# One maximum unit of thirteen half passes moved from the place in front of the eighth score unit to that in front of the seventh

## What is computed

```python
q_pool = q.reshape(B, H, S // factor, factor, D).mean(axis=3)     # B=4, H=8, S=1152, D=64, factor=2
scores = scale * np.matmul(q_pool, k.transpose(0, 1, 3, 2))
scores = scores - np.max(scores, axis=-1, keepdims=True)
attn = np.exp(scores)
attn = attn / (np.sum(attn, axis=-1, keepdims=True) + 1e-09)
return np.matmul(attn, v).astype(np.float32)
```

## Time and profile before

| | |
|---|---|
| time, median of 3 runs (lowest, highest) | 917.2 us (916.99, 917.43) |
| the profiled execution, its own time | 918.22 us |
| span of that execution | 916.2 us |
| outside the span | 2.0 us |
| PE, PEld busy | 884.3 us (97%), 717.6 us (78%) |
| DVE, ACT, POOL busy | 545.8 us (60%), 470.6 us (51%), 387.3 us (42%) |
| granted TensorE clock, mean of the span | 0.995 |

### The profile page before, as it was taken

The page is one execution under the profiler, slowest core; times in us unless marked ns, Lnnn a source line. Parts: engine busy times, 40 slices in busy tenths (PEclk is TensorE's granted clock), DMA queues, the critical chain, the costliest instruction groups (busy, mean ns, idle before and its releaser), DMA issues.

```text
span 916.2 us, 18068 instructions
## 1 busy us (share of the span) xinstructions
PE 884.3 (97%) x7190; PEld 717.6 (78%) x7190; DVE 545.8 (60%) x971; ACT 470.6 (51%) x1017; POOL 387.3 (42%) x269
## 2 busy tenths in 40 slices
PE   4899999999999999998999999999999999999996
PEld 3566666676676666665999999999999999999733
DVE  6878888888888888853664434433433443443423
ACT  3677787877777777686543322322332332322202
POOL 3979999999999999997000000000000000000000
PEclk9999999999999999999999999999999999999998
DMA  7121122222212211303320000200000000476998
GB/s 237 39 75 55 51 79 79 79 79 78 69 63 80 79 50 56 97 1 117 115 69 1 1 1 0 93 1 1 1 1 1 1 1 1 168 244 219 302 369 286
DMA packets 47828, 76.42 MB, mean 83 GB/s; under 512 B 3584, under 2 KB 33408, under 8 KB 47744
## 3 DMA queue, kind: packets, MB, share of 16 engines
q1 hardware_dynamic: 47744, 75.26, 24.5%
HBM read 70.53 MB, written 4.72 MB: 82 GB/s over the span
## 4 chain that ended last, share of the span: by engine, by line
PE 54%; issue 26%; POOL 16%; DVE 2%; ACT 1%; DMA 0%; POOLq 0%; ACTq 0%
POOL acc L1555 11%; PE psum L684 8%; PE psum L686 7%; PE psum L685 7%; PE psum L666 7%; PE psum L668 7%; PE psum L667 7%; POOL acc_early L1555 5%; PE psum L834 2%; PE psum L811 2%; DVE mx L1186 1%; PE psum L620 1%; PE psum L858 1%; PE psum L724 1%; PE psum L704 1%
## 5 line engine op out<-in xcount | busy, mean ns | idle before, releaser
L948 ACT ACTIVATE pt<-psum 128x576 f32<-128x576 f32 x288 | 174.4, 649 | 77.5 <-PE psum L607 77.4
L1186 DVE TENSOR_REDUCE mx<-psum 128x1 f32<-128x512 f32 x256 | 162.4, 678 | 51.4 <-PE psum L570 51.2
L620 PE MATMUL psum<-pt,vs 128*64 128x288 f32 x1152 | 153.6, 412 | 0.0
L1555 POOL TENSOR_TENSOR acc<-acc,pt 128x576 f32<-128x576 f32 x94 | 148.6, 1581 | 0.3 <-ACT pt L948 0.3
L1390 DVE TENSOR_SCALAR gf<-gf 128x384 f32<-128x384 f32 x96 | 34.5, 360 | 190.5 <-ACT gf L1102 190.5
L1102 ACT ACTIVATE gf<-psum 128x384 f32<-128x384 f32 x96 | 47.2, 492 | 196.0 <-PE psum L668 195.4
L684 PE MATMUL psum<-gh,W 128*128 128x384 f32 x384 | 131.9, 344 | 0.0
L685 PE MATMUL psum<-gl,W 128*128 128x384 f32 x384 | 128.5, 335 | 0.0
L686 PE MATMUL psum<-gh,W 128*128 128x384 f32 x384 | 128.5, 335 | 0.0
L666 PE MATMUL psum<-xh,W 128*128 128x384 f32 x384 | 128.4, 334 | 0.0
L668 PE MATMUL psum<-xh,W 128*128 128x384 f32 x384 | 128.3, 334 | 0.0
(11 more groups left out here) (171 smaller groups left out, 2060.0 us busy)
## 6 DMA issues: line engine op xcount, KB each, us to landing
ring<-in_w SPq DMA_DIRECT2D x62, 512.0 KB, 5.9
vs<-in_v SPq DMA_DIRECT2D x16, 576.0 KB, 3.8
kraw<-in_kT SPq DMA_DIRECT2D x15, 576.0 KB, 3.7
qraw<-in_qT SPq DMA_DIRECT2D x15, 576.0 KB, 4.7
out<-ob SPq DMA_DIRECT2D x18, 256.0 KB, 3.6
wst<-in_w_in SPq DMA_DIRECT2D x16, 256.0 KB, 2.7
wst<-in_w_out SPq DMA_DIRECT2D x16, 256.0 KB, 3.2
spare_half<-in_w SPq DMA_DIRECT2D x2, 512.0 KB, 7.5
```

The costliest lines, as they stand in the source:

```text
L620: ins = mm(psum[64 * s:64 * s + 64, O_BANK, 0:HALF], vs[:, p % NB, s, kt * D:(kt + 1) * D], pt[:, i % NPT, s, :], start=(kt == 0), stop=(k ...
L948: act.activation(pt[:, i % NPT, :, :], t_pair(("T", h, kt))[:, :, 0:HALF], ACT.Exp, scale=SCALE)\
L1186: dve.tensor_reduce(mx[:, b, u // 2, s, u % 2:u % 2 + 1], bank, AX.X, ALU.max).then_inc(s_red, 1)
L1555: pool.tensor_tensor(to, one, other, ALU.add).then_inc(s_acc, 1)
```

## The change

In even half passes with h of 4 or more, U5 of the next pair moves from key 7 of the table to key 6. It applies where the next pair exists: h = 4, 6, ..., 28, thirteen half passes. Nothing is added or removed.

```diff
--- before.py
+++ after.py
@@ -211,7 +211,7 @@
         elif h == 2:
             units = {0: ((1, 1),), 2: ((1, 2),), 3: ((1, 3),), 4: ((1, 4),), LATE: ((1, 9),), 7: ((1, 5),), END: ((1, 6),)}
         elif h % 2 == 0:
-            units = {0: ((1, 2),), 2: ((1, 3),), 4: ((1, 4),), LATE: ((1, 9),), 7: ((1, 5),), END: ((1, 6),)}
+            units = {0: ((1, 2),), 2: ((1, 3),), 4: ((1, 4),), LATE: ((1, 9),), 6: ((1, 5),), END: ((1, 6),)}
         else:
             units = {0: ((1, 7),), 2: ((1, 8),), 4: ((1, 10),), LATE: ((2, 0),), 7: ((2, 1),)}
```

## The result

The changed kernel takes 926.04 us (median of 4 runs, 925.47 to 927.01) against 917.19 us. It is slower, by 8.85 us. The ratio estimated from all the runs is 1.0093, interval 1.0081 to 1.0105; the quotient of the two medians, 1.0096, lies inside it. The forecast of 921.8 us had the sign, but its 4.6 us are little more than half of the loss, and the time lies outside the range.

A forecast was written before the change was run, and what follows sets the result against it. TensorE, with the exponentials it waits for, was taken to bound the kernel; 13 x 0.35 = 4.55 us of delay on a median of 917.2 us gave 921.8 us, with an 8 in 10 range of 919.3 to 923.4 us.

The forecast's parts named there:

- What bounds the kernel: In the attention's half passes, TensorE with the exponentials it waits for sets the pace; GpSimd follows with 1.26 us slack per pair.
- GpSimd's idle: In each pair of half passes, GpSimd's slack grows by 0.35 us, to 1.6 us idle.
- the rival that it holds the pace: GpSimd's additions set the pace, so a delay of T8 vanishes and the time stays 917.2 us; chance 0.07.
- The even half pass: U5 ahead of T6 delays E6, T8 then waits for E6, and the products with v come 0.35 us later.
- The wait for the bank: U5 waits for VectorE's reduction of U9's first bank, starting at 108.91 instead of 108.89 us: almost no cost.
- The last step: From U6 to the products with v in the even half pass: 111.36 to 111.76 us, 0.40 us.
- The term of the sum: Delay of the products with v in each of thirteen even half passes: 0.35 us.
- everything they wait for later was itself started by TensorE, so the delay passes on whole: Behind U6, into the odd half pass, the 0.35 us delay is neither earned back nor enlarged.
- E5: Exponential of tile 5, in the even half pass from 109.12 to 109.77 us; GpSimd's addition of tile 5 waits for it.
- the rival of a falling clock: TensorE's extra short waits in thirteen half passes lower its clock: 40 us lost, 957 us; chance 0.02.
- The forecast of the gain: Rival: the maximum stream runs ahead, saving at most 1.4 us at U6 and T8: 915.8 us; chance 0.03.
- VectorE took the reciprocal first: In the even half pass, VectorE's reciprocal from 109.34 to 110.38 precedes U5's reduction, which stays at 110.30 to 110.93 us.

The follow-up runs named there:

- 4: Kernel before, with four VectorE memsets of 128x64 ahead of L1266 and a GpSimd memset of 128x320 in odd half passes 5 to 27: 917.22 us.
- 3: Kernel before, with four VectorE memsets of 128x64 ahead of L1266 in odd half passes 5 to 27: 925.32 us.
- 7: Changed kernel, with a GpSimd memset of 128x128 between the first and second addition of odd half passes 5 to 27: 927.70 us.
- 6: Kernel before, with two VectorE memsets of 128x64 ahead of L1266 in odd half passes 5 to 27: 925.22 us.

## Why the prediction was half right

**What bounds the kernel** was right: TensorE with the exponentials. GpSimd's idle grew, as forecast in kind (0.95 + 0.31 us to 1.39 + 1.15 us in a pair, where 1.6 us was forecast), and the rival that it holds the pace fell.

**The even half pass** was right step by step: U5 0.71 us behind T5 (0.65 said), T6 1.01 (0.99), T7 1.56 (1.57), E6 1.77 (1.75), T8 2.47 (2.46), U6 3.11 (3.10), L620 3.44 us (3.50). The wait for the bank cost 0.08 us, where 0.02 was allowed. The last step was 0.33 us instead of 0.40, since U6 no longer waits and its weights come early. The term of the sum was 0.35 us and measured 0.30. Where it stands alone, with GpSimd 0.3 us later, it gives 921.09 us; the forecast was 921.8 us.

**The step that failed** is "everything they wait for later was itself started by TensorE, so the delay passes on whole". The delay did pass on, but GpSimd was not part of what passed it on. The prediction counted GpSimd only as an engine that TensorE might wait for. It has slack there, but its additions and VectorE's two-input work in SBUF exclude each other without any semaphore (the text ahead of the prediction has the engines meet only through semaphores, and so did the prediction), and its phase comes from E5, ahead of the delay. So the change slid VectorE 0.31 us against GpSimd, over a lead of 0.09 us. The missing term: L1266 1.05 us longer (0.75 to 1.80 us), of which VectorE's idle of 0.38 us ahead of the reduction and TensorE's own slack took a part; the unit in front of T7 0.59 us later; T7 1.97 instead of 1.47 us behind T5; 0.10 us given back because T7 no longer waits for E5 and T8 follows it in 0.53 instead of 0.63 us; 0.38 us in the mean of twelve half passes, 4.6 us.

It could have been read before: the additions of 1.92 and 1.94 us among others of 1.42, and L1261 at 1.96 us in odd and 1.13 to 1.18 us in even half passes 6 to 26, are an engine held by another (even the 1.18 us were partly a hold: in the even half passes 6 to 26 of the changed kernel L1261 takes 0.74 to 0.77 us), on VectorE's path to a bank that TensorE takes just in time. The Trainium skill, SBUF — State Buffer, section "Who interferes with whom", states the rule: a VectorE instruction with two SBUF inputs contends with a GpSimd instruction that reads SBUF, and the order of issue decides who is blocked. The runs agree, in both orders: L1266 0.75 us and the addition 1.92 us with L1266 first, 1.80 and 1.40 us with the addition first. A prediction that had asked of each two-input instruction of VectorE who gets there first would have found that a slide of 0.35 us is greater than the lead of 0.09 us, and put a term there. That it would have had its size of 4.6 us right is not shown.

**The clock** stayed at 1.00 in these half passes, so the rival of a falling clock did not occur. The forecast of the gain (915.8 us) did not either: VectorE took the reciprocal first, as said.

## What to carry to other kernels

When an engine is delayed, ask not only who waits for it, but which engines slide against each other: those timed from ahead of the delay and those timed from behind it. Where two of them share something exclusive, here VectorE and GpSimd with two-input work in SBUF, look for the smallest lead in the trace of before. Once a shift has used that lead up, how late the held engine comes no longer counts (VectorE 0.15 us later cost as much as 0.3 us), but when the other's instruction ends does: the stall here was anything from 0.04 to 0.58 us in a half pass. Where the lead is kept, lateness cost nothing. A place in which one unit fills another's wait is free once; its neighbours on both sides are not.

## What was not expected of the hardware

How long L1266 is held follows from the addition under way, to 0.01 us. Not held, it takes 0.69 us (in 4). It ends 0.62 us after that addition's end in the changed kernel (118.40 + 1.40 = 119.80 and 118.62 + 1.80 = 120.42 us), in 3 (119.50 and 120.12 us), in 7 (120.16 and 120.78 us) and, for 6, 0.61 us after it (119.88 and 120.49 us). Even in the kernel before it ends 0.62 us after the end of the first addition (116.86 + 1.42 = 118.28 and 118.90 us): it came in the last 0.13 us of that one, and ahead of the second. The profile shows such a hold as a longer instruction, not as idle time, on either engine.

Not all work takes a turn. VectorE's reciprocal, with one input in SBUF, took 1.04 us before, beside an addition of 1.43 us. A memset on either engine took none: GpSimd's took 0.37 to 0.38 us beside VectorE's work, and four of VectorE's together 0.33 us beside an addition of 1.41 us.
